# The last down projection of a three-layer kernel as seven block products, with weight sums kept in device memory

## The reference

```python
def _moe2_ref(x, w_in, w_out):     # x 2304 x 512, w_in 512 x 2048, w_out 2048 x 512
    h = x @ w_in
    r = np.maximum(h, 0.0)
    g = r * r
    return (g @ w_out).astype(np.float32)
```

## Time and profile before

| | |
|---|---|
| median of 3 runs | 881.88 us |
| profiled execution | 882.57 us, of which span 880.8 us |
| PE busy | 864.2 us (98%) |
| DVE / ACT / POOL busy | 546.8 / 468.2 / 541.8 us |
| last run's down stage (chunk 0 to the last matmul) | 810.07 to 877.84 us |
| down stages of runs 3 and 4 | their last matmuls end at about 628.1 and 753.0 us |

### The profile page before, as it was taken

The page is one execution under the profiler, slowest core; times in us unless marked ns, Lnnn a source line. Parts: engine busy times, 40 slices in busy tenths (PEclk is TensorE's granted clock), DMA queues, the critical chain, the costliest instruction groups (busy, mean ns, idle before and its releaser), DMA issues.

```text
span 880.8 us, 16629 instructions
## 1 busy us (share of the span) xinstructions
PE 864.2 (98%) x6436; PEld 852.2 (97%) x6436; DVE 546.8 (62%) x617; ACT 468.2 (53%) x990; POOL 541.8 (62%) x521
## 2 busy tenths in 40 slices
PE   7898999999999999999999999999999999999998
PEld 6687999999999999999999999999999999999998
DVE  4759676558567548755557677676477674577222
ACT  5877665645565644555555455444455443554332
POOL 3746398583589665388856368563386743585332
PEclk9989999999999999999999999999999999999999
DMA  8863122222222212222222222222422222420222
GB/s 277 264 205 100 49 73 72 61 61 60 84 73 72 67 54 60 78 73 73 73 65 60 72 73 73 60 60 71 146 72 73 60 60 61 153 75 26 54 66 96
DMA packets 87007, 75.01 MB, mean 85 GB/s; under 512 B 5520, under 2 KB 70032, under 8 KB 86928
## 3 DMA queue, kind: packets, MB, share of 16 engines
q1 hardware_dynamic: 86784, 73.65, 28.1%
q10 hardware_dynamic: 144, 0.29, 0.1%
HBM read 69.21 MB, written 4.72 MB: 84 GB/s over the span
## 4 chain that ended last, share of the span: by engine, by line
PE 94%; DVE 3%; ACT 1%; issue 1%; POOL 1%; DVEq 0%; POOLq 0%
PE banks L732 30%; PE banks L734 30%; PE banks L733 30%; PE banks L691 1%; PE banks L633 1%; ACT probs L1004 1%; DVE probsT L1244 1%; PE banks L705 1%; DVE acts L1184 0%; PE banks L665 0%; DVE banks L1224 0%; PE banks L641 0%; DVE neg_max L1231 0%; PE banks L713 0%; PE banks L697 0%
## 5 line engine op out<-in xcount | busy, mean ns | idle before, releaser
L732 PE MATMUL banks<-xc_hi,w_hi 128*128 128x384 f32 x844 | 282.7, 335 | 0.2 <-DVE xc_lo L1216 0.2
L734 PE MATMUL banks<-xc_hi,w_lo 128*128 128x384 f32 x844 | 281.9, 334 | 0.0
L733 PE MATMUL banks<-xc_lo,w_hi 128*128 128x384 f32 x844 | 281.9, 334 | 0.0
L584 POOL TENSOR_TENSOR d_lo<-d_raw,d_hi 128x512 fp32r<-128x512 f32 x84 | 127.3, 1516 | 174.8 <-ACT d_hi L935 174.8
L732 PE MATMUL banks<-hs_hi,d_hi 128*128 128x384 f32 x672 | 225.1, 335 | 0.1
L734 PE MATMUL banks<-hs_hi,d_lo 128*128 128x384 f32 x672 | 224.5, 334 | 0.0
L733 PE MATMUL banks<-hs_lo,d_hi 128*128 128x384 f32 x672 | 224.5, 334 | 0.0
L1322 DVE TENSOR_TENSOR hs_lo<-h,hs_hi 128x768 fp32r<-128x768 f32 x84 | 86.4, 1028 | 137.4 <-ACT hs_hi L935 137.2
L732 PEld LDWEIGHTS banks<-xc_hi,w_hi 128*128 128x128 f32 x844 | 158.5, 188 | 0.6 <-DVE xc_lo L1216 0.4
L733 PEld LDWEIGHTS banks<-xc_lo,w_hi 128*128 128x128 f32 x844 | 158.5, 188 | 0.0
L734 PEld LDWEIGHTS banks<-xc_hi,w_lo 128*128 128x128 f32 x844 | 158.4, 188 | 0.0
(11 more groups left out here) (93 smaller groups left out, 1074.5 us busy)
## 6 DMA issues: line engine op xcount, KB each, us to landing
d_raw<-in_w_down SPq DMA_DIRECT2D x48, 256.0 KB, 2.6
w_raw<-in_w_gate SPq DMA_DIRECT2D x36, 256.0 KB, 2.9
w_raw<-in_w_val SPq DMA_DIRECT2D x72, 128.0 KB, 2.8
d_raw<-in_w_out SPq DMA_DIRECT2D x36, 256.0 KB, 2.6
v_sb<-in_v_rows SPq DMA_DIRECT2D x16, 384.0 KB, 5.0
w_raw<-in_w_in SPq DMA_DIRECT2D x24, 256.0 KB, 2.7
w_raw<-in_w_in SPq DMA_DIRECT2D x48, 128.0 KB, 2.7
q_sb<-in_qT SPq DMA_DIRECT2D x16, 288.0 KB, 4.7
```

What stands on the lines that cost most here:

```text
L584: nc.gpsimd.tensor_tensor(d_lo[m % 2][:], d_raw[m % 2][:], d_hi[m % 2][:].bitcast(F32), ALU.subtract).then_inc(dlo_done, 1)
L732: pe.matmul(ps, w_h, v_h, start=first, stop=False, skip_group_check=joined)
L733: pe.matmul(ps, w_h, v_l, start=False, stop=False, skip_group_check=joined)
L734: return pe.matmul(ps, w_l, v_h, start=False, stop=last, skip_group_check=joined)
```

## The change

The down stage of the last run (r = 5) becomes seven block products. The 16 chunks are taken as 8 pairs (even, odd); with the two halves of the output rows and the two column halves this is a 2x2 block product. A product takes all 8 pairs: each pair is a *part* of 6 matmuls, two parts are a *duo*. 7 products x 4 duos = 28 duos = 56 parts = 336 matmuls, in the order P1, P7, P6, P2, P5, P4, P3. Before, the stage had 16 x 24 = 384.

The seven weight blocks (A11, A12, A22 and the sums S1 to S4, high and low parts) are made in the down stages of runs 3 and 4, four pairs of chunks in each: pairs at f = (2,3), (6,7), (8,9), (12,13). Run 4 goes through its chunks in the order 2, 3, 0, 1, 6, 7, ..., so that its four pairs are the other four. For each such pair POOL makes four sums of 128x256 (`kept_sums`), ACT rounds them in two copies of 128x512 (`kept_high`), DVE makes two low parts (`kept_low`), and SP stores the pair and its sums to a device-memory tensor `stash` in six transfers (`keep_chunk`). The load into a `d_raw` buffer now also waits for the sums that read it, and `down_high`/`down_low` wait for the stores that read `d_hi`/`d_lo` (`free_kept`). Some preparations of the next run move: POOL's weight sums from f = 1,2,3,4 to 2,3,4,6, ACT's `high1`/`high2` one chunk later, the splits of T1 and B22 to f = 14 and 15.

In the last stage SP loads one 256 KB weight tile for each part from `stash` (ring of 6). ACT and DVE round and split the operand of each duo, 128x768 (ring of 6 duos, `duo_high`, `low_duo`). The sums of `h` are made in place: T1, T2, T4 by POOL, T3 by DVE, four instructions of 128x768 each.

The core of the diff:

```diff
+D_ORDER = ("P1", "P7", "P6", "P2", "P5", "P4", "P3")
+KEEPING = (LAST - 2, LAST - 1)
+KEPT_AT = (1, 3, 4, 6)
             def load_d(m):
                 if m >= 2:
                     sp.wait_ge(dlo_done, m - 1)
...
+                    if k is not None:
+                        sp.wait_ge(s_kept, 4 * (k + 1))
+            def keep_chunk(r, f):
...
+                sp.wait_ge(dhi_done, m + 1)
+                sp.wait_ge(dlo_done, m + 1)
...
+                if odd:
+                    sp.wait_ge(s_kept_hi, 2 * (k + 1))
+                    sp.wait_ge(s_kept_lo, 2 * (k + 1))
+            def load_kept(e):
...
+                if e >= W_RING:
+                    sp.wait_ge(part_done, e - W_RING + 1)
+                sp.dma_start(w_kept[:, e % W_RING, :].bitcast(F32),
+                             stash[bass.ds((D_WEIGHT[D_ORDER[n]] * PARTS + j) * P, P), :]).then_inc(kept_in[e % W_RING], 16)
             def down_low(m):
                 pool.wait_ge(dhi_done, m + 1)
+                free_kept(pool, m)
+            def kept_sums(r, k):
...
+                nc.gpsimd.tensor_tensor(s1, a21, a22, ALU.add).then_inc(s_kept, 1)
+                nc.gpsimd.tensor_tensor(s3, a11, a21, ALU.subtract).then_inc(s_kept, 1)
...
+                nc.gpsimd.tensor_tensor(s2, s1, a11, ALU.subtract).then_inc(s_kept, 1)
...
+                nc.gpsimd.tensor_tensor(s4, a12, s2, ALU.subtract).then_inc(s_kept, 1)
+            h_t1(0)
+            h_a(U0[RUNS] - 1, LAST)
+            h_t1(1)
+            h_b(U0[RUNS] - 1, LAST)
+            h_t1(2)
+            h_t1(3)
+            for i in range(DUOS):
+                h_t2(i)
+            for i in range(DUOS):
+                h_t4(i)
             def down_high(m):
...
+                free_kept(act, m)
+            low_duo(2)
+            h_t3(0)
+            low_duo(3)
+            for i in range(1, DUOS):
+                h_t3(i)
+                low_duo(3 + i)
```

More of the change, by code:

```diff
@@ L322, in raw_part, with h_duo, duo, result @@
             return w_raw[u % 2][:, n * HALF_K:(n + count) * HALF_K]
+        def h_duo(product, i):
+            odd, c = D_BLOCK[product]
+            return h[:].rearrange("p (j o c t) -> p j o c t", o=2, c=2, t=NT)[:, 2 * i:2 * i + 2, odd, c, :]
+        def duo(t, e):
+            n = e % H_RING
+            return two(t[:, n * PW:(n + 1) * PW])
+        def result(row, c):
+            return half_cols(LAST, row, c)
+        x_banks = [u_banks(LAST)[3], u_banks(LAST)[2]]
+        z_banks, y_banks = v_banks(LAST)[0:2], v_banks(LAST)[2:4]
+        at = X_T1 * PW
+        kept_hi, kept_lo = xc_hi[:, at:at + 2 * D], xc_lo[:, at:at + 2 * D]
+        kept_sum = [kept_raw[n // 2][:, n % 2 * HALF_K:(n % 2 + 1) * HALF_K] for n in range(4)]
         def output(g, run):
@@ L607, in _ @@
                         down_low(m + 1)
+                    if f % 2 == 1 and kept(r, f + 1) is not None:
+                        kept_sums(r, kept(r, f + 1))
                     if f == 0:
@@ L927, in _, with part @@
                     down(m, r, 1)
+            def part(e, j, row, banks, fresh):
+                n = e * 2 + j
+                w, x = n % W_RING, n % PARTS
+                pe.wait_ge(kept_in[w], 16 * (n // W_RING + 1))
+                rows_ = slice(row * P, (row + 1) * P)
+                low = slice(HALF_K + row * P, HALF_K + (row + 1) * P)
+                return three(banks[row][:, 0:NT], w_kept[:, w, rows_], w_kept[:, w, low],
+                             duo(xc_hi, e)[:, j, :], duo(xc_lo, e)[:, j, :],
+                             fresh and x == 0, x == PARTS - 1, not fresh)
+            for n, product_ in enumerate(D_ORDER):
+                banks = {"P2": z_banks, "P7": y_banks, "P4": y_banks}.get(product_, x_banks)
+                fresh = product_ in ("P1", "P7", "P2")
+                if product_ == "P1":
+                    pe.wait_ge(c11_done, steps_done(U0[RUNS] - 1))
+                    pe.wait_ge(c21_done, steps_done(U0[RUNS] - 1))
+                if product_ == "P6":
+                    pe.wait_ge(p1_out, 2)
+                if product_ == "P5":
+                    pe.wait_ge(p6_out, 2)
+                if product_ == "P4":
+                    pe.wait_ge(p7_kept, 2)
+                if product_ == "P3":
+                    pe.wait_ge(r22_done, 2)
+                for i in range(DUOS):
+                    e = n * DUOS + i
+                    pe.wait_ge(duo_lo, e + 1)
+                    if e < 7 * DUOS - 1:
+                        for j in range(2):
+                            for row in range(2):
+                                mm = part(e, j, row, banks, fresh)
+                            mm.then_inc(part_done, 1)
+                    else:
+                        for row in range(2):
+                            for j in range(2):
+                                mm = part(e, j, row, banks, fresh)
+                            mm.then_inc(rows_done, 1)
+                    if e == 0:
+                        p3(U0[RUNS] - 1, LAST)
         @block.scalar
@@ L1375, in _ @@
                         h_low(m + 1)
+                    if f % 2 == 0 and kept(r, f) is not None:
+                        kept_low(kept(r, f))
                     if q < RUNS:
```

234 lines of the change are left out of this document (218 added, 16 removed).

## The result

| | before | after |
|---|---|---|
| median (4 runs each) | 882.36 us (881.54 to 883.51) | 896.27 us (894.59 to 896.81) |
| ratio after/before | | 1.0154, 95% interval 1.0134 to 1.0173 |
| profiled execution, span | 880.8 us | 895.1 us |
| down stage of run 3 | 67.7 us | 75.9 us |
| down stage of run 4 | 67.7 us | 75.7 us |

The stages are read from PE's start times: a stage's first matmul to the first of what follows, or to the last one plus its pitch. They add up: +8.2 and +8.0 in the keeping stages, -2.9 in the last, and 1.0 us that the attention part was longer in this execution, before anything that was changed: 14.3 us, the difference of the two spans. The stretches between the stages and the tail are within 0.1 us of what they were.

A forecast was written before the change was run, and what follows sets the result against it. PE, busy 98% of the span, was taken as the bound. -8.3 + 2 x 6.7 + 5.5 = +10.6 us gave 893.2 on the profiled execution, 892 as median; range 880 to 896.5 us.

The forecast's parts named there:

- the two places: Where PE would wait: the down stages of runs 3 and 4, 6.7 us each, and the last stage's start, 5.5 us.
- the forecast case: Whole kernel: PE waits in keeping stages and at the last stage's start, time 886 to 894 us; chance 0.62.
- the transfers: Rival: in keeping stages even chunks' stores must land before ACT overwrites them; 896 us, band over 894, chance 0.10.
- The 48 matmuls, -8.3 us: Last down stage: 384 - 336 = 48 matmuls fewer at 0.173 us each, saving 8.3 us.
- POOL and DVE exclude each other: DVE instructions with two SBUF inputs and POOL instructions reading SBUF run in turn; a 0.94 us DVE sum takes 2.05.
- DVE instructions which read a bank take no part: Such DVE instructions stay outside the exclusion with POOL: `va` takes its 0.56 us within the same stretch.
- The keeping stages, 6.7 us each: Down stages of runs 3 and 4: PE waits for POOL's low parts, 6.7 us a stage, 2.8 to 8.4.
- its warning: Keeping-stage stores: completion may come late for device memory; a microsecond more would take the stage to the high end.
- its high end of 8.4: Keeping stage: 8.4 us of cost if each transfer lands at 3.0 us and moves at 250 GB/s.
- The start of the last stage, 5.5 us: Last stage, duos 3 to 6: PE 5.5 us late for low parts behind POOL's and DVE's sums; ends 0 and 6.0.
- The loads of the last stage, 0: Last stage: weight loads, 252 GB/s needed, cost PE 0; at 250 GB/s all told it would be 2 us.
- Hidden: Rival: sums, splits and stores fit beside PE in all three stages; 873.6 us, band under 880, chance 0.14.

The follow-up runs named there:

- e4_small_t: Changed kernel with the last stage's sums T1 to T4 made over 8 of 384 columns only; 890.83 us, 1.0089 of the kernel before.
- e10_all: Changed kernel with one kept pair, even-chunk stores and next-run preparations moved, plus the last-stage order of e7_reordered; 878.45 us, 0.9946 of the kernel before.
- e2_no_sums: Changed kernel without the kept pairs' sums, ACT copies and DVE low parts, all stores still made; 880.80 us, 0.9980 of the kernel before.
- e7_reordered: Changed kernel with the last stage's products in the order P1, P2, P3, P7, P6, P5, P4; 890.23 us, 1.0099 of the kernel before.
- e8_both: e7_reordered plus pair (8,9) moved to (10,11), even-chunk stores ahead of a load, POOL's last weight sums later; 884.89 us, 1.0030 of the kernel before.
- e3_no_stores: Changed kernel with nothing stored in the keeping stages and no waits for stores, sums still made; 892.48 us, 1.0102 of the kernel before.

## Why the prediction was right, and where it was off

The direction, the two places and the mechanism were right. That the range held is in part luck: 896.27 lies outside the forecast case (886 to 894), in the band to which the transfers had been given 0.10, and 0.2 us inside the range. The profiled execution lost some 1.7 us in two stretches of a lower clock, which no term of the forecast holds; how often the other executions had them is not known, and one of them took 896.76 us at a mean granted clock of 0.994, that of the kernel before.

**The 48 matmuls, -8.3 us.** Right: without its pauses (e4_small_t, e10_all) the last stage is 60.6 us against 67.6, and the rest, 1.3 us, is one wait and the restart of PE. The working has a slip that changes nothing: from 810.07 to 877.50 there are 389 steps, not 383, since six matmuls of the last up product stand in the stage, so this too gives 0.173 us and not 0.176.

**POOL and DVE exclude each other.** Right, and it is the cause of nearly everything. The rows above show it at every turn, and e2_no_sums and e4_small_t take the shared time away and the pauses with it. The whole trace of the changed kernel bears it out: in 334 places a TENSOR_TENSOR row of DVE that reads no bank overlaps one of POOL by more than 0.2 us, and in none do the two end less than 0.54 us apart, which is the shortest time that the forecast gave for holding (0.56, a low part of 128x512). If they shared the time instead of taking turns, some would end together. No kernel was run in which only the exclusion is taken away.

That DVE instructions which read a bank take no part was read from a row that does not show it: `va` starts at 809.23, after POOL's row beside it had ended (807.41 + 1.54 = 808.95). The trace of the changed kernel does show it:

```profile
649.78 0.74 POOL L604 TENSOR_TENSOR w_raw<-w_raw 128x256 f32<-128x256 f32 x1
649.78 0.56 DVE L1655 TENSOR_TENSOR va<-banks,c_u 128x384 f32<-128x384 f32 x1 [0.48 <-PE banks L912]
```

Both start at once, and neither takes longer than alone.

**The keeping stages, 6.7 us each: right in kind, 1.4 us short.** Late starts of chunks in run 3, forecast and measured:

| chunk | 3 | 4 | 5 | 6 | 7 | 8 | 9 | 10 | 14, 15 |
|---|---|---|---|---|---|---|---|---|---|
| forecast | 0.45 | 1.04 | 0.68 | 0.22 | 0.50 | 1.04 | 2.02 | 0.88 | 0 |
| measured | 0.66 | 0.95 | 0.63 | 0.14 | 0.76 | 0.96 | 2.12 | 1.70 | 0.36 |

Two terms were too small. Each pause costs PE some 0.1 us more than the wait, since the matmul after it starts late as well (0.28 us behind the first instead of 0.17). And the 1.70 at chunk 10 is no wait: after the pause of 1.8 us the granted clock, the share of full speed at which PE may run, is 0.53 for 3.5 us, which is the lower of its two levels, and 11 matmuls start 0.32 us apart instead of 0.17. The windows before and at that place:

```profile
596.00:605.80 9.80, 7.42 (x42) 6.78 (x40) 7.64 (x7) 3.19 (x6) 8.89 (x7) 1.00 0.59 194
606.00:609.60 3.60, 3.60 (x12) 3.60 (x13) 3.60 (x5) 1.97 (x3) 0.13 (x1) 0.53 0.76 242
```

The trace of e7_reordered settles its price, since its keeping stages are the same code: there the clock stays at 1.00 after a pause of the same length, chunk 10 is late by 0.74 and chunk 11 by 0.14, together the forecast 0.88, and the stages are 75.0 and 74.9 instead of 75.9 and 75.7. So the low clock costs 0.8 to 0.9 us a stage, in the executions that have it. It is what the forecast left out; the forecast's own terms were short by some 0.6 us a stage.

**The stores.** The forecast let the stores of chunk 2, for which chunk 4's `d_hi` waits, land 2.7 us after issue. The stores in the view of run 3's keeping stage (number, size, median us to landing):

```profile
stash<-d_hi SPq DMA_DIRECT2D x4, 128.0 KB, 2.7
stash<-d_lo SPq DMA_DIRECT2D x4, 128.0 KB, 2.8
stash<-d_lo SPq DMA_DIRECT2D x4, 256.0 KB, 4.5
```

and ACT waited for it as said:

```profile
577.92 0.63 ACT L1156 ACTIVATE d_hi<-d_raw 128x512 fp32r<-128x512 f32 x1 [1.90 <-DMA stash<-d_lo]
```

So it is at chunks 8 and 10, by 0.94 and 1.42 us (and by 0.3 to 0.4 at chunks 5 and 9). The stores of even chunks, 128 KB, land in 2.7 and 2.8 us, as the forecast assumed. Those of odd chunks, 256 KB and issued one behind the other, take 4.1 and 4.5, and the loads of 256 KB in the same stage a median 3.7 us where they took 2.6 before; how much of that is the queue and how much the writing was not separated, and no matmul waited for a load there. (The section of the Trainium skill that the forecast named for its warning describes transfers that GpSimd issues; these are issued by SP.) The warning's price was also mis-added: by the forecast's own rule, 0.1 us of PE at three pairs a stage for each 0.1 us of landing, a microsecond more gives 6.7 + 3.0 = 9.7 us a stage, above its high end of 8.4. The rival in which transfers decide was wrong as a mechanism, though the time came out beside its 896: e2_no_sums has all the stores and no wait.

**The start of the last stage, 5.5 us.** Measured 5.4: four pauses of some 1.35 us of PE's time each, of which the view of waits counts 1.0 to 1.1. The four duos are the ones named.

**The loads of the last stage, 0.** Right: in the changed kernel no row of PE waits for them. Of the four traces without the pauses, two show one wait for a load (1.0 us in e4_small_t, 0.4 in e7_reordered) and two none (e8_both and e10_all, with the last stage of e7_reordered). So the loads are close to being late, but that they must show once the pauses are gone is not so.

**The rivals.** "Hidden" rested on the busy shares (36 and 27 us of 50), which had room. They are the wrong measure for two engines that cannot work at once. Their sum, 63 of 50, is no measure either: that stage ran without a wait of PE, because the rows include the time in which one engine waits for the other. What has to be summed is the time for which each instruction holds what they share, as the forecast's count did for chunks 1 to 9: 31.3 of 37.4 us before, 41.9 after.

## What to carry to other kernels

When work is to be hidden beside TensorE on VectorE and GpSimd, add their times for instructions that read two tiles, each time taken where the instruction ran alone, and compare the sum with the time there is; then look at each chunk, since a stage that has room in total (here 61 of 67 us) may have none where two kinds of work meet. Before a scheme with fewer products is given up, move the preparations to the chunks that are free, issue a store ahead of a load that has to wait, and put the products without operand sums first: here almost the same instructions went from 896 to 878 us by such moves (in the traces 1.7 us of it were the lower clock).

## What the runs showed of the hardware that was not expected

After a pause of 1.8 us at the end of a stretch with several pauses, PE's granted clock fell to its lower level for some 3.5 us in both keeping stages of the changed kernel's trace (0.53) and of e4_small_t's, and stayed at 1.00 in the same stages, with the same code, of e7_reordered. After pauses of 1.5 us (e3_no_stores) and less it never fell in these stages. What decides it stays open.

Stores of 14.7 MB to device memory over two stages, beside their loads, left no trace in PE's time (e2_no_sums: 178 GB/s at a share of 0.57, PE busy 67.00 of 67.00 us).
